# Who issues the stores and where a batch's way back and table end, in a fused FFT convolution and mixture-of-experts kernel

## The reference

```python
X = np.fft.rfft(x, axis=1)                    # x: (8, 3072, 256) float32
y = np.fft.irfft(X * (filt_r + 1j * filt_i)[None], n=3072, axis=1)
x = y.reshape(8 * 3072, 256)
logits = x @ w_gate                           # 8 experts
expert_idx = np.argmax(logits, axis=1)
probs = np.exp(logits - logits.max(-1, keepdims=True)); probs /= probs.sum(-1, keepdims=True) + 1e-9
# in token order, each expert takes its first 768 tokens; the others give zeros
h = np.maximum(np.einsum('ecd,edf->ecf', disp, w1), 0.0)      # w1: (8, 256, 1024)
out[i] = gate_w[i] * (h @ w2)[expert_idx[i], pos[i]]          # w2: (8, 1024, 256)
```

## The kernel before

| stage | steps (3) of batch | first transform of | way back of | routing of |
|---|---|---|---|---|
| 0 | 0 | batch 1, from h = 8 | none | none |
| 1 | 1 | batch 2, from h = 0 | batch 0, token step h - 4 | none |
| 2 | 2 | none | end of batch 0 (h = 0 to 3), batch 1 (h - 3) | batch 0, steps by `STEPS_BY` |
| close | none | none | last three token steps of batch 1, then all of batch 2 | end of batch 0, then batch 1 |

## Time and profile before

### The profile page before, as it was taken

The page is one execution under the profiler, slowest core; times in us unless marked ns, Lnnn a source line. Parts: engine busy times, 40 slices in busy tenths (PEclk is TensorE's granted clock), DMA queues, the critical chain, the costliest instruction groups (busy, mean ns, idle before and its releaser), DMA issues.

```text
span 587.5 us, 9953 instructions
## 1 busy us (share of the span) xinstructions
PE 466.5 (79%) x4008; PEld 382.2 (65%) x4008; DVE 262.8 (45%) x390; ACT 203.4 (35%) x342; POOL 219.2 (37%) x187
## 2 busy tenths in 40 slices
PE   3154756688879857568974499999999999999995
PEld 1032332245435533348974489999999999999995
DVE  7246544255466857666830263225341244422220
ACT  2201322344334424344310164425453345443320
POOL 9150100000000000075347425775676764866312
PEclk9668977799998977578998599999999999999999
DMA  8899997978796659569931130692308913194001
GB/s 311 301 375 418 368 302 227 318 231 250 229 256 209 193 147 259 187 214 399 378 112 45 45 99 28 238 388 82 126 28 309 362 45 118 34 359 175 19 28 41
DMA packets 65368, 121.26 MB, mean 206 GB/s; under 512 B 7984, under 2 KB 35360, under 8 KB 64160
## 3 DMA queue, kind: packets, MB, share of 16 engines
q1 hardware_dynamic: 40656, 69.31, 35.8%
q10 hardware_dynamic: 15632, 25.87, 13.7%
q0 software_dynamic: 9024, 25.34, 11.9%
HBM read 60.69 MB, written 59.81 MB: 205 GB/s over the span
## 4 chain that ended last, share of the span: by engine, by line
PE 60%; DVE 10%; issue 9%; ACTq 6%; DMA 6%; ACT 6%; SPq 1%; POOL 1%; POOLq 0%; DVEq 0%
PE back L1125 21%; PE wide L1111 12%; PE high L1111 11%; PE back L385 6%; DMA x_in<-in_x 4%; DVE pq L656 3%; ACTq L532 3%; PE low L1094 2%; PE wide L372 2%; ACT v_out L549 2%; PE low L423 1%; SPq L532 1%; DMA y_rows<-y 1%; ACTq L554 1%; ACT t_out L538 1%
## 5 line engine op out<-in xcount | busy, mean ns | idle before, releaser
L1125 PE MATMUL back<-w2h,hh 128*128 128x256 f32 x384 | 109.9, 286 | 1.0 <-ACT o_out L896 1.0
L1125 PE MATMUL back<-w2l,hh 128*128 128x256 f32 x384 | 108.6, 283 | 0.0
L1125 PE MATMUL back<-w2h,hl 128*128 128x256 f32 x384 | 108.6, 283 | 0.0
L938 DVE SCALAR_TENSOR_TENSOR hl<-wide,hh 128x384 fp32r<-128x384 f32 x64 | 34.6, 555 | 132.6 <-ACT hh L887 105.3
L656 DVE TENSOR_TENSOR pq<-wide,fab 128x1024 f32<-128x1024 f32 x48 | 58.8, 1224 | 75.8 <-PE wide L372 75.8
L1029 POOL DMA_INDIRECT out<-o_out,token x48 | 52.2, 1087 | 83.0 <-ACT o_out L896 72.3
L1001 POOL DMA_INDIRECT g_in<-y_rows,token x48 | 51.5, 1073 | 65.7 <-DVE token L810 43.6
L1125 PEld LDWEIGHTS back<-w2h,hh 128*128 128x128 f32 x384 | 73.5, 192 | 1.4 <-ACT o_out L896 1.2
L1125 PEld LDWEIGHTS back<-w2l,hh 128*128 128x128 f32 x384 | 73.6, 192 | 0.0
L1125 PEld LDWEIGHTS back<-w2h,hl 128*128 128x128 f32 x384 | 73.6, 192 | 0.0
L372 PE MATMUL wide<-z_in,wf 64*64 64x256 f32 x384 | 34.2, 426 | 37.9 <-DVE pq L656 23.5
(11 more groups left out here) (129 smaller groups left out, 831.3 us busy)
## 6 DMA issues: line engine op xcount, KB each, us to landing
out<-zero SPq DMA_DIRECT2D x24, 1024.0 KB
w_raw<-in_w SPq DMA_DIRECT2D x16, 1024.0 KB
u_scratch<-v_out ACTq DMA_DIRECT2D x48, 192.0 KB, 3.6
y_rows<-y ACTq DMA_DIRECT2D x36, 256.0 KB, 4.1
v_in<-u_scratch SPq DMA_DIRECT2D x30, 256.0 KB, 5.5
z_in<-t_scratch SPq DMA_DIRECT2D x24, 256.0 KB, 3.8
x_in<-in_x POOLq DMA_DIRECT2D x6, 1024.0 KB, 14.0
x_in<-in_x SPq DMA_DIRECT2D x3, 1024.0 KB, 6.9
```

The costliest lines, as they stand in the source:

```text
L938: nc.vector.scalar_tensor_tensor(out=hl[:, b % 2, f, :], in0=ps[(2, 3, 6, 7)[f % 4]][:, 0:TOK], scalar=0.0, in1=hh[:, b % 2, f, :].bitcast ...
L1125: mm = nc.tensor.matmul(ps[4 + (b * ST + s) % 2][:, 0:D], hx[:, b % 2, f, s * P:(s + 1) * P], wt[:, k, f, :], start=(f == 0 and m == 0), s ...
```

## The change

Six things:

- *Stores of t.* The first stage's 12 are shared: half a = 0 by ScalarE right after its copy, half a = 1 by SyncE. Those of batches 1 and 2 are issued by GpSimd, with batch 2's x loads in between (`x_load` of part m after stores c = 2m and 2m + 1). The first stage has semaphores of its own (`t_first`).
- *Stores of y.* All by GpSimd (`rows_out`): in the stages after the t stores, in the close five pairs before the first gather and the sixth behind the second gather.
- *Start.* GpSimd loads the second quarter of the tables before it waits for the first stores; the five constants are issued by ScalarE before stage 0.
- *Batch 1's way back* ends in stage 2: from h = 13 on two token steps in each step (`CLOSE_FROM`, `ai_steps`), 10 to 15.
- *Batch 0's table* is made at h = 13 of stage 2, into a free part of bank 7, and before step 14's inverse TensorE waits until VectorE has added it (`TABLED`). `STEPS_BY` brings the routing steps forward: 28 of 30 by h = 12 instead of 24, and the last two at h = 13. The close holds nothing of batch 0 or of batch 1's tokens.
- *Rows in the close*: after steps 21, 22, 23, 24, 25 instead of 16, 18, 21, 23, 25.

```diff
-TABLE_STEP = 1
+TABLE_STEP = 13
+CLOSE_FROM = 13
-ROWS_AFTER = [16, 18, 21, 23, 25]
+ROWS_AFTER = [21, 22, 23, 24, 25]
-STEPS_BY = [0, 0, 0, 3, 7, 9, 12, 14, 16, 18, 20, 22, 24, 26, 27, 28]
+STEPS_BY = [0, 0, 0, 3, 7, 9, 12, 15, 18, 22, 24, 26, 28, 30, 30, 30]
...
+        def ai_steps(h, ai, ai_from, closing):
+            if ai is None or h < ai_from:
+                return []
+            if closing and h >= CLOSE_FROM:
+                i = CLOSE_FROM - ai_from + 2 * (h - CLOSE_FROM)
+                return [i, i + 1]
+            return [h - ai_from]
...
         def pe_stage(...):
                 pe_forward(pe, t, r, h)
-                if after_another and h == TABLE_STEP:
-                    pe.wait_ge(v_evac, t * NG)
-                    pe_table(pe, rt - 1, 4)
+                if rt is not None and h == TABLE_STEP + 1:
+                    pe.wait_ge(route_step, rt * ROUTE_STEPS + TABLED)
...
-                if ai is not None and h >= ai_from:
+                for i in ai_steps(h, ai, ai_from, a is None):
...
                 if rt is not None and h == ai_from + RANK_STEP:
                     pe_rank(pe, rt, 7)
+                if rt is not None and h == TABLE_STEP:
+                    pe_table(pe, rt, 7)
...
-        def pe_last(pe, t, before):
-            for i in range(NH - before, AI_SPAN):
-                pe_tokens(pe, t - 1, i, t + 1, False)
+        def pe_last(pe, t):
             pe.wait_ge(v_evac, (t + 1) * NG)
-            pe_table(pe, t - 2, 4)
...
         def act_a(act, t, c):
...
-            if t not in (0, FIRST):
-                act.wait_ge(t_evac, t * NCH + c + 1)
-                t_store(act, t, c)
+            if t in (0, FIRST):
+                t_store(act, t, c, 0)
...
-            if 2 <= i < 14 and i % 2 == 0:
-                act_rows_out(act, t, i // 2 - 1)
...
         def dve_last(dve, t, r):
...
-            for n in range(HOT, ROUTE_STEPS):
-                dve_route(dve, t - 2, n, 4)
             for n in range(HOT):
                 dve_route(dve, t - 1, n, 4)
...
         def pool_last(pool, t, r):
             gate_store(pool, t - 1)
+            for c in range(NCH - 1):
+                rows_out(pool, t, c, True)
...
                 pool_gather(pool, r, 0)
                 low_split(pool, r, 0, 1)
                 pool_gather(pool, r, 1)
+                rows_out(pool, t, NCH - 1, True)
...
                 load_tables(pool, 1)
+                t_stored(pool, first)
+                pool.nop(nofuse=True)
                 load_tables(pool, 2)
...
                 def stage(t, a, a_from, ai, ai_from, before, rt):
-                    if a is not None and a + 1 < last:
-                        for m in range(NM):
-                            x_load(pool, a + 1, m)
-                    if rt is not None:
-                        gate_store(pool, rt)
+                    if a is not None:
+                        for c in range(NCH):
+                            for k in range(2):
+                                t_store(pool, a, c, k)
+                            if a + 1 < last and c % 2 == 1:
+                                x_load(pool, a + 1, c // 2)
+                    for c in range(NCH):
+                        if ai is not None:
+                            rows_out(pool, ai, c, False)
+                        if rt is not None and c == 2:
+                            gate_store(pool, rt)
```

More of the change, by code:

```diff
@@ L304, in z_load @@
             if g == 0:
-                for i in range(3):
-                    sp.wait_ge(t_written[i], (t + 1) * 64)
+                t_stored(sp, t)
             if n >= ZB:
@@ L613, in act_stage, with act_last @@
             act_back(act, t, NG - 1)
-        def act_last(act, t, r, before):
-            for i in range(NH - before, AI_SPAN):
-                act_tokens(act, t - 1, i, False)
+        def act_last(act, t, r):
             for i in range(AI_SPAN):
@@ L661, in dve_stage @@
                     dve_fold(dve, nxt, h - (NH - 2))
-                if ai is not None and 0 <= h - ai_from < 12 and (h - ai_from) % 2 == 0:
-                    dve_rows(dve, ai, (h - ai_from) // 2, False)
-                if after_another and h == TABLE_STEP:
-                    for step in range(HOT, ROUTE_STEPS):
-                        dve_route(dve, rt - 1, step, 4)
+                for i in ai_steps(h, ai, ai_from, a is None):
+                    if i < 12 and i % 2 == 0:
+                        dve_rows(dve, ai, i // 2, False)
                 if rt is not None:
@@ L1196, in run @@
                 for c in range(NCH):
[L1197 to L1199 removed]
+                    t_store(sp, first, c, 1)
                 sp.wait_ge(gaps_set, r + 1)
```

113 lines of the change are left out of this document (63 added, 50 removed).

## The result

The changed kernel takes 596.17 us (median of 4 runs, 593.43 to 597.14) beside 587.34 us (4 runs) for the kernel before: a ratio of 1.0129, 95% interval 1.0078 to 1.018. It is slower by about 1%, which is clear of the interval; I had forecast 569 us. Its profiled execution took 596.57 us, with a span of 594.7. In a second set of runs the ratio was 1.0085 (1.0053 to 1.0117).

A forecast was written before the change was run, and what follows sets the result against it. Waits bound the kernel before 345 us, TensorE's own matmuls after. Terms 0 - 5 - 6 - 3 + 4 - 8 = -18 us, off the 587.1 us median, gave 569 us; own range 562 to 576, overall 554 to 582.

The forecast's parts named there:

- part 1: Opening: shared first stores, with early tables and constants beside them, net 0 us (from -2 to +4).
- half of it falls into the time in which the engines now stand: Opening: of 6.5 us of table and constant transfer, half fits idle engine time, so stores land up to 3 us later.
- part 2: Rest of stage 0: ScalarE's store issues and the waits they cause go, -5 us (-9 to -1).
- What is late next is a transfer: Rest of stage 0: 11.7 MB at 390 GB/s, then 5 us until z is in, puts product 17 at 86.5 us.
- rival A: Front bound by its transfers: t stores on GpSimd's queue wait behind x and tables; 577 us, chance 0.20.
- part 3: Start of stage 1: constants and twelve t issues leave ScalarE, -6 us (-8 to -2).
- Rival C: GpSimd's stores land late at stage 1's z and the close's fourth row pair; slower, up to 593 us, chance 0.06.
- part 4: Stage 2: the y_rows issues leave ScalarE, -3 us (-5 to 0); nothing in steady stage 1.
- part 5: Stage 2: batch 1's last steps and batch 0's table move in, costing +4 us (+2 to +7).
- rival D: Stage 2: the table waits for late routing steps and delays the way back, costing 12 us; 577 us, chance 0.07.
- part 6: Close, from last inverse to expert part: 42 us instead of 50, -8 us (-11 to -3).
- Rival B: Expert part: TensorE's stall between 308 and 334 us, some 17 us, goes too; 552 us, chance 0.10.

The follow-up runs named there:

- u_t: The changed kernel with the t stores of batches 1 and 2 on ScalarE's queue again: ratio 1.0001 to the kernel before.
- mix3_xlast: mix3 with GpSimd issuing batch 2's x loads behind all t stores of batch 1 instead of between them: ratio 0.9928 to the kernel before.
- u_cast: The changed kernel with ScalarE's w2 copy at token step 9 of the close instead of 6: ratio 0.9907 to the kernel before.
- after_again: The changed kernel, unaltered, in a second set of runs: ratio 1.0085 to the kernel before.
- mix3: The changed kernel with its whole opening as before and the w2 copy at token step 9: ratio 0.9882 to the kernel before, 0.9849 when repeated.
- o_consts: The changed kernel with the constants issued after stage 0 again: ratio 1.0162 to the kernel before.

## Why the prediction was wrong, point by point

**The opening** (part 1, 0, from -2 to +4) was +5.5 in the profile, +4.8 between the means: above the bound. The step that failed is "half of it falls into the time in which the engines now stand" and with it the 3 us allowed for the stores. The last issue did come earlier, by 1.6 us (20.62 instead of 22.24), as forecast. But the stores shared the engines with the tables, and the last one, on which all of stage 0 waits, took 7 us longer to land (3.67 to 10.39) and was there 5.1 us later, not 3. I had seen 416 GB/s as the price and not asked who is served last.

**Rest of stage 0** (part 2, -5) was 0: 58.2 us from z0 to z1 in 4 profiles with the stores on ScalarE and the old opening, 58.4 in 4 of the changed code. The ScalarE waits went, and in their place the last t store took 14.68 us to land, and TensorE stood 9.11 us for z. I had it in the sentence "What is late next is a transfer", but priced it at bandwidth, with 5 us from the last byte to z: that is the step that failed. With the opening undone the stretch gives 0.3 us (57.9, 4 profiles, from 56.6 to 61.1), and with the changed opening it is shorter with the stores left on ScalarE (54.3, u_t). This is near rival A, to which I gave 0.20: product 17 came after 96 us, beyond its mark of 90, though 5.5 us of that are the opening's. Its condition, t stores that wait behind x and tables in one queue, is not all of the cause, since mix3_xlast with x behind them starts stage 1 no earlier.

**Start of stage 1** (part 3, -6) was right by its own measure, -6.6 to the first product. It was no gain, since 3.5 us of it were paid back by the fourth: loads of v and z that take 11 to 14 us, and in a smaller part the y buffer that waits for a t store. Rival C named this (stores of GpSimd that land late where they are waited for) but at the z loads and in the close, not at the first copy of y rows. Its end, +6, is near the measured +7 to +9, but by chance: it wanted landings of 17 to 20 us at both places, z's store took 14.68, and in the close no copy waited over 5 us for a y store.

**y stores** (part 4, -3, from -5 to 0) hold: -1.5 in the old order, -3.1 in the new, the latter from one profile with them on ScalarE.

**New order in stage 2** (part 5, +4, from +2 to +7) holds: +4.4 (+6.0 with the y stores on ScalarE, one profile). The mark for rival D, over 4 us of idle TensorE at step 14, didn't show.

**The close** (part 6, -8) was +2.1, and here lies the largest miss, 10 us. The sum of it was sound for VectorE: with the w2 copy at step 9 the close is 45.2 us, 7 less than before. The step that failed is the list of what stands between the last inverse and the transposes: it left out the w2 copy. The kernel before had it at 240.65 us, 31.6 us after its last inverse, waiting 2.39 us; I had not put that row in the sum. Shortening everything around it made it the bound: the weights, issued behind the v loads, come at +33.2 us in the changed kernel, and ScalarE waited 8.66 us for them; the fifth y copy, its rows, the last two large steps and the table stand behind. "It is +23" at the fourth pair was met (240.01 for its copy); the next copy, which was to follow some 3 us later, came at 252.20.

**The end**: 323.6 to 328.3 us from the transposes in the ten profiles without a star, 326 forecast. An earlier start may give some of it back (328.3 for u_cast, which begins at 256.0, and 323.6 for the changed kernel, which begins at 271.1), but after_again has 328.1 from 266.3, so this isn't shown.

Put together with the forecast's own terms: opening +5, stage 0 0 instead of -5, start of stage 1 up to the fourth product -3 instead of -6, y stores and order +5 between there and the last inverse where -3 and +4 stood, close +2 instead of -8, the end -2.5: +7 instead of -18. The +5 holds the gain of the y stores as well: by the means above, order and y stores together are +2.9 (79.2 against 76.3 us). The rest is this profile's own, 80.8 us, and what it comes from isn't shown; the second profile of the same code has 79.7.

The four single undoings (opening 0.8%, t stores 0.8%, order 1.2%, w2 copy 1.8% below after_again) add up to much more than the 0.9 to 1.3% that were lost. So they are not terms of a sum: each is what one part costs while the others are there.

## What to carry to other kernels

When a chain of waits is shortened, list every instruction of the in-order engines in the new, shorter stretch that waits for a transfer, and write down when that transfer lands, counted from the same start: a copy that waits 2 us today and has no share in the path is the next bound. Ask also behind which issues of its own queue that transfer stands. Moving stores to another queue freed the issuing engine and nothing else here; with the DMA engines busy nine tenths of the time, the stores landed later (9 to 17 us against 5 to 6), and a buffer that is shared with the next stage waited for them. Early transfers were not free because the engines stood idle later: the small stores that were queued beside them paid. And test a forecast's parts on the kernel before as well: the one line that mended the change also brought the old order, written in the change's code, to the same ratio.

## What the runs showed that I had not expected

**The stall in the expert part goes with the chip or the hour, not with the change.** Rival B left open whether the 17 us that TensorE loses between 308 and 334 us hang on the burst of indirect DMAs or on the queues. On the three chips of the starred spans it is gone in all ten profiles, and GpSimd issues the same indirect DMAs at the same pace of 1.3 us. TensorE's busy time, clock and the rest from 300 to 345 us in the changed kernel (second profile), then in mix3:

```profile
300.00:345.00 45.00, 25.67 (x168) 23.72 (x167) 8.38 (x19) 5.65 (x13) 24.19 (x24) 0.75 0.22 70
```

```profile
300.00:345.00 45.00, 43.20 (x283) 42.60 (x283) 20.39 (x32) 21.73 (x38) 35.35 (x29) 0.96 0.21 68
```

The two windows don't hold the same work, as mix3's transposes come 15 us earlier; o_consts, with its transposes at 270.3, has TensorE busy 39.68 of the 45 us at a clock of 0.96. From the transposes to the end it is 305.2 to 307.2 us there, 20 us less, and the kernel before, unaltered, has a median of 568 us. So the cause is not in an edit. The starred runs are also the later ones, and their chips are not the one of the earlier variants, so whether it is the chip or the time stays open, and so does the mechanism.

**A landing time is a matter of company.** The same 256 KB in 1 KB pieces landed in 3.7 us in the opening of before, 10.4 us there beside tables, 14.7 us on GpSimd's queue and 5.9 on ScalarE's (u_t), both beside x and u; y rows of the close went from 3.8 us to 6.4 us. The prices of the earlier trace rows held only for the traffic in which they were read. The Trainium skill, DMA: Bandwidth & Descriptors, Specifications, gives about 1 us to the first byte on GpSimd's path and about 0.6 on the others; no run here shows that apart from the queueing.
